# Gate logits of a routed expert layer from one pass over weights of 16 columns, six matrix products for a block in place of nine

## The chip, the cores and the metric

The kernel runs on one core of one Trainium2 chip. The metric is the time on the device in microseconds (us); lower is better. Times are medians of several executions, and one further execution was taken with the hardware profiler.

## The reference

The program is three layers one behind the other. The attention runs over 32 (batch, head) pairs with 768 tokens each; then comes a layer of eight experts, whose routing weights are made from gate logits by an exponential and eight rounds of normalisation over rows and columns; then a gated layer of two products. Only the middle one touches the change:

```python
def _moe_ref(x, w_gate, w1, w2):          # x: 3072 x 384, w_gate: 384 x 8
    logits = x @ w_gate
    logits = logits - logits.max()
    P = np.exp(logits)
    for _ in range(8):
        P /= P.sum(1, keepdims=True) + 1e-09
        P /= P.sum(0, keepdims=True) + 1e-09
        P *= N / E
    out = np.zeros((N, D), dtype=np.float32)
    for e in range(E):
        h = np.maximum(x @ w1[e], 0.0)
        ye = h @ w2[e]
        out += P[:, e:e + 1] * ye
    return out.astype(np.float32)
```

## The kernel before

Big matrix products are made in the type float32r, which TensorE takes in one product, from operands that are split into a high half (the value rounded to that type) and a low half (what the rounding left). A full product is then three: high by high, high by low, low by high. `PARTS = ((0, 0), (0, 1), (1, 0))` names them as (half of the weights, half of x). With the depth of 384 in three pieces of 128 (`KC` = 3) that makes nine matrix products of 384 columns for each output tile of a block of `TB` = 384 tokens. The 3072 tokens are eight such blocks, 0 to 7.

The program has two parts. In the first (the attention) the loop `for p in BODIES` goes over 24 pairs of (batch half, chunk of 128 tokens), and each body writes out by hand the order in which TensorE works: level products (L418, L428, L432, in the wait chain called `level_y` and `level_x`), the chain of the recurrence (L444, L456, L465, L473, L483 to L491), and between them eight slots, filled by the table `slots(p)`. A slot holds a tile of the expert layer's first product (`early_products`, L200), a turn of a finished tile of x (L499), or, always in slot 6, the gate logits: at p = 4, 7, ..., 19 the products of block 0 to 5 (`logit_products`, L509), and in the body behind each (p = 5, 8, ..., 20) their turn (`logit_flip`, L518). The products leave the logits of a block as 8 rows by 384 tokens in a bank of the accumulator memory (tile `bank`); VectorE copies them to `logit_a` (L826); the turn makes three tiles of 128 tokens by 8 experts of them with TensorE's transpose; and ScalarE copies these to `logit` (L641). TensorE, and every other engine, does its instructions in program order and waits on counters (semaphores) of the others. Since the accumulator banks of the slots are shared, the first product of a slot waits for the copy of the slot before the last.

The second part begins at about 606 us with the last six tiles of x. There the gate logits of blocks 6 and 7 are made in the same way (`logits_t`, L1219; `logits`, L1228; VectorE's copy L1445, ScalarE's copy L1353). The tile `gated`, in whose first rows that copy lands, shares its memory with `h_raw` and is shown under that name. Then come the maximum (L1502, L1256, L1504, L1260, L1506), the exponential (L1373) and the eight rounds of normalisation (VectorE L1511 to L1529 with one TensorE product each, L1328). TensorE fills the time with more tiles of the first expert product (L200), whose weights GpSimd (POOL) splits in L254. From 665 us on TensorE does the expert products one behind the other (L1292, L1321).

The gate weights are split once, by VectorE in `gate_split`, ahead of body p = 3.

Of the kernel before, what the change touches and what calls it, by code (L numbers as in the profile page):

```python
# [23 lines left out]
F32 = mybir.dt.float32  # L24
F32R = mybir.dt.float32r
F16 = mybir.dt.float16
BF16 = mybir.dt.bfloat16
ALU = mybir.AluOpType
# [3 lines left out]
P = 128  # L32
# [4 lines left out]
TB = 384  # L37
SINKHORN = 8
IDENT, UPPER, FIRST_T, LEVEL = 0, 1, 2, 2
PARTS = ((0, 0), (0, 1), (1, 0))  # L40
# [14 lines left out]
def wait(eng, sem, value):  # L55

    if isinstance(value, int) and value <= 0:
        return
    eng.wait_ge(sem, value)
# [41 lines left out]

def build(nc, kq_rows, kv_cols, beta_cols, w_gate, w1, w2, w_in, w_out, masks, out):
    NG, NCH, _, _, GH, D = kv_cols.shape
    S = NCH * P
    HS = beta_cols.shape[2]
    DM = w_gate.shape[0]
    KC = DM // P
    E, F = w1.shape[0], w1.shape[2]
# [10 lines left out]
    PASSES = early_passes(E * NH)  # L119
    EARLY_OF = [(i, hn, b, f) for i, (hn, blocks) in enumerate(PASSES) for b in blocks for f in range(FC)]  # L120
    PASS_FIRST = [FC * sum(len(blocks) for _, blocks in PASSES[:i]) for i in range(len(PASSES) + 1)]
    EARLY = len(EARLY_OF)
    IN_ATTENTION = (PAIRS - EARLY_FROM) * UPS
# [6 lines left out]
    with ExitStack() as top:  # L130
        def sb(name, shape, dt=F32, ctx=top):
            return ctx.enter_context(nc.sbuf_tensor(name, shape, dt))
# [4 lines left out]
        bank = top.enter_context(nc.psum_tensor("bank", [P, 8, 512], F32))  # L137


        ident = sb("ident", [P, P])  # L140
# [3 lines left out]
        x_early = sb("x_early", [P, 2, KC, EARLY_TOK], F32R)  # L144
# [2 lines left out]
        route = sb("route", [P, NT, E])  # L147
        logit = sb("logit", [P, NT, E])
        gate_raw = sb("gate_raw", [P, KC, E])
        gate_hl = sb("gate_hl", [P, 2, KC, E], F32R)  # L150
        rowsum = sb("rowsum", [P, NT])
        colsum = sb("colsum", [P, E])
        top1 = sb("top1", [P, 4])
# [22 lines left out]
        pe_xx, act_hi, dve_lo, dve_gate = map(sem, ("pe_xx", "act_hi", "dve_lo", "dve_gate"))  # L176
        pe_lt, dve_lt, pe_logit, act_logit = map(sem, ("pe_lt", "dve_lt", "pe_logit", "act_logit"))
# [34 lines left out]
        def early_store(sp, n):  # L212
            _, hn, blk, f = EARLY_OF[n]
            sp.wait_ge(act_e, n + 1)
            sp.dma_start(h_early[hn, blk, f, :, :], h_out[:, n % RING, :]).then_inc(st_h[n % RING], 16)
# [42 lines left out]
        with ExitStack() as at:  # L258
# [29 lines left out]
            logit_a = sb("logit_a", [P, TB], ctx=at)  # L288
# [59 lines left out]
            with nc.Block() as block:  # L348
# [47 lines left out]
                def _(pe):  # L396
# [106 lines left out]
                    def logit_products(b, to):  # L503

                        pe.wait_ge(dve_t, TT * (b + 1))
                        pe.wait_ge(dve_gate, 2)
                        for n, (a, c) in enumerate(PARTS):
                            for kc in range(KC):
                                m = pe.matmul(bank[0:E, to, 0:TB], gate_hl[:, a, kc, :],  # L509
                                              x_early[:, c, kc, b * TB:(b + 1) * TB], start=n + kc == 0,  # L510
                                              stop=n == len(PARTS) - 1 and kc == KC - 1)
                        m.then_inc(pe_lt, 1)

                    def logit_flip(b, to):

                        pe.wait_ge(dve_lt, b + 1)
                        for t in range(TT):
                            m = pe.transpose(bank[:, to, t * E:(t + 1) * E], logit_a[0:E, t * P:(t + 1) * P],  # L518
                                             ident[0:E, 0:E])
                        m.then_inc(pe_logit, 1)  # L520

                    def body(p):
                        ser, dbl, pre = pair(p), pair(p + 1), pair(p + 2)

                        def early(at, parts=range(9)):

                            if (item := slots(p)[at]) is None:
                                if -1 <= p < EARLY_FROM and at < 4:
                                    for _ in range(BUSY):
                                        pe.matmul(bank[:, BE + 1, 3 * P:4 * P], ident16[:, :], ident16[:, :],  # L530
                                                  start=True, stop=True)
                                return
                            if 0 in parts and (last := slot_before(p, at)) is not None:
                                done = {"up": act_e, "turn": dve_t, "logit": dve_lt, "flip": act_logit}[last[0]]
                                pe.wait_ge(done, last[1] + 1)
                            if item[0] == "up":
                                early_products(pe, item[1], BE + at % 2, parts)
                            elif item[0] == "turn":
                                turn_early(item[1], BE + at % 2)
                            elif item[0] == "logit":  # L540
                                logit_products(item[1], BE + at % 2)
                            else:
                                logit_flip(item[1], BE + at % 2)
# [168 lines left out]
                def _(dve):  # L712
# [109 lines left out]
                    def logits_out(b, at):  # L822
                        dve.wait_ge(pe_lt, b + 1)

                        wait(dve, pe_logit, b)
                        dve.tensor_copy(logit_a[0:E, :], bank[0:E, at, 0:TB]).then_inc(dve_lt, 1)  # L826

                    def gate_split():
                        dve.wait_ge(ld_gate, 16)
                        dve.tensor_copy(gate_hl[:, 0, :, :], gate_raw[:, :, :]).then_inc(dve_gate, 1)  # L830
                        dve.wait_ge(dve_gate, 1)
                        dve.tensor_tensor(gate_hl[:, 1, :, :], gate_raw[:, :, :], gate_hl[:, 0, :, :].bitcast(F32),
                                          ALU.subtract).then_inc(dve_gate, 1)

                    def body(p):
                        late, ser, dbl, pre, nrm = pair(p - 1), pair(p), pair(p + 1), pair(p + 2), pair(p + 3)

                        def early(at):

                            item = slots(p)[at]  # L840
                            if item is not None and item[0] == "turn":
                                turned_low(item[1], BE + at % 2)
                            if item is not None and item[0] == "logit":
                                logits_out(item[1], BE + at % 2)
# [47 lines left out]
                    for p in BODIES:  # L892
                        if p == -1:
                            dve.wait_ge(act_id, 1)
                        if p == EARLY_FROM - 1:
                            gate_split()
                        body(p)
# [110 lines left out]
        sig, gated = h_raw[:, 0:2, :], h_raw[:, 2:4, :]  # L1008
        w1_next = w1_raw[len(PASSES) % 2]
        w2_next = w_raw[:, 1 - len(PASSES) % 2, :].rearrange("p (k n) -> p k n", k=FC)  # L1010
        BL, BM, BL_T = 4, 5, 6
        logit_t = gated[0:E, :, :]
        out_t = out.rearrange("(t p) n -> p t n", p=P)
        EARLY_UNITS = {(hn, b) for hn, blocks in PASSES for b in blocks}
        HALVES = E * NH + NQ
# [3 lines left out]
        def x_at(c, kc, first, n):  # L1019

            if first < EARLY_TOK:
                return x_early[:, c, kc, first:first + n]
            return x_late[:, c, kc, first - EARLY_TOK:first - EARLY_TOK + n]
# [48 lines left out]
        with nc.Block() as block:  # L1072
# [132 lines left out]
            def _(pe):  # L1205
# [8 lines left out]

                def logits_t(b):
                    pe.wait_ge(dve_lo, TT * (b + 1) - ET)
                    for n, (a, c) in enumerate(PARTS):
                        for kc in range(KC):
                            m = pe.matmul(bank[0:E, BL_T + b % 2, 0:TB], gate_hl[:, a, kc, :],  # L1219
                                          x_at(c, kc, b * TB, TB), start=n + kc == 0,  # L1220
                                          stop=n == len(PARTS) - 1 and kc == KC - 1)
                    m.then_inc(pe_lt, 1)

                def logits(b):
                    pe.wait_ge(dve_lt, b + 1)
                    wait(pe, act_logit, b)
                    for t in range(TT):
                        m = pe.transpose(bank[:, BL, t * E:(t + 1) * E],  # L1228
                                         logit_t[:, b % 2, t * P:(t + 1) * P], ident[0:E, 0:E])
                    m.then_inc(pe_logit, 1)  # L1230

                def early(n):
# [9 lines left out]
                turn(21)  # L1242
                early(BEFORE_MAX[1])
                logits_t(6)
                turn(22)
                turn(23)
                early(BEFORE_MAX[2])
                logits(6)
                early(BEFORE_MAX[3])
                logits_t(7)  # L1250
                early(BEFORE_MAX[4])
                logits(7)
# [73 lines left out]
                for n in range(SINKHORN):  # L1326
                    pe.wait_ge(dve_sink, 3 + 8 * n + 4)
                    pe.matmul(bank[:, BM, 0:NT * E], ones[:, :], route.rearrange("p t e -> p (t e)"),  # L1328
                              start=True, stop=True).then_inc(pe_sink, 1)
# [105 lines left out]
            def _(dve):  # L1435
# [6 lines left out]

                def logits_out(b):
                    dve.wait_ge(pe_lt, b + 1)
                    dve.tensor_copy(logit_t[:, b % 2, :], bank[0:E, BL_T + b % 2, 0:TB]).then_inc(dve_lt, 1)  # L1445

                for t in range(18, 22):
                    turned_low(t)
# [59 lines left out]
                for n in range(SINKHORN):  # L1508
                    at = 3 + 8 * n
# [62 lines left out]
```

## Time and profile before

| | us |
|---|---|
| median of 3 runs (lowest, highest) | 2451.62 (2451.11, 2452.88) |
| the profiled execution, its own time | 2452.09 |
| its span in the profile | 2450.3 |
| TensorE busy with products | 2401.2 (98%) |
| VectorE, ScalarE, GpSimd busy | 1005.2, 659.3, 823.8 |

The span is the time from the first to the last instruction that the profile shows. The records of products overlap: each is shown from its start to its modelled end, so the cost of a product in a row of them is the distance from one start to the next, not the duration of a record. In the timeline a row merges like instructions: start, length from the first start to the last end, engine, line, operation, operands, count, and in brackets the idle time before it.

### The profile page before, as it was taken

The page shows a single profiled execution, that of the slowest core. Times are in us where ns is not written, and L with a number is a line of the kernel's source. Part 1 is how long each engine was busy: PE and PEld are TensorE (multiplying, and loading weights), DVE is VectorE, ACT ScalarE, POOL GpSimd, SP SyncE. Part 2 cuts the span into 40 slices and gives each one's busy share as a digit, 9 for nine tenths or more (in the row PEclk, how much of TensorE's full clock was granted, in tenths as well). Part 3 has the DMA queues.
Part 4 walks back from the last instruction along what each step waited for, and adds up shares of the span by engine and source line. Part 5 has one row for each costly group of instructions (what it writes and reads, how often), then busy time and mean ns, then how long its engine had stood idle before and what let it go on. Part 6 is the DMA issues. An engine that isn't in the chain of part 4 may idle for free.

```text
span 2450.3 us, 41885 instructions
## 1 busy us (share of the span) xinstructions
PE 2401.2 (98%) x17603; PEld 2329.4 (95%) x17603; DVE 1005.2 (41%) x2165; ACT 659.3 (27%) x1445; POOL 823.8 (34%) x831
## 2 busy tenths in 40 slices
PE   5999999999899999999999999999999999999999
PEld 4888888888899999999999999999999999999999
DVE  4866666664533333333333333333333343333332
ACT  3444444444321112111111111111111123222222
POOL 4655454542331333312302311321230413453432
PEclk9999999999999999999999999999999999999999
DMA  2233333322311111101110110110111100000001
GB/s 98 73 119 111 112 110 116 108 90 95 116 65 46 33 52 65 52 2 51 52 39 14 52 39 14 52 52 3 50 52 39 52 27 14 14 27 1 1 20 59
DMA packets 83963, 134.01 MB, mean 55 GB/s; under 512 B 5568, under 2 KB 62144, under 8 KB 83776
## 3 DMA queue, kind: packets, MB, share of 16 engines
q1 hardware_dynamic: 83776, 131.33, 16.2%
q8 instruction: 140, 2.29, 0.4%
q14 instruction: 47, 0.39, 0.0%
HBM read 98.28 MB, written 33.03 MB: 54 GB/s over the span
## 4 chain that ended last, share of the span: by engine, by line
PE 74%; DVE 1%; issue 0%; ACT 0%
PE bank L1321 41%; PE bank L1292 32%; PE bank L200 1%; PE bank L1268 0%; DVE rowsum L1513 0%; PE bank L1328 0%; PE bank L1219 0%; DVE route L1529 0%; PE bank L1211 0%; DVE route L1517 0%; DVE rowsum L1511 0%; ACT h_out L210 0%; DVE rowsum L1515 0%; DVE colsum L1521 0%; PE bank L1228 0%
## 5 line engine op out<-in xcount | busy, mean ns | idle before, releaser
L1321 PE MATMUL bank<-w_hl,h_hl 128*128 128x384 f32 x5760 | 1018.2, 334 | 0.0
L1321 PEld LDWEIGHTS bank<-w_hl,h_hl 128*128 128x128 f32 x5760 | 1000.2, 188 | 0.0
L1292 PE MATMUL bank<-x_early,w_hl 128*128 128x384 f32 x3024 | 539.1, 334 | 0.7 <-ACT h_out L210 0.7
L1292 PEld LDWEIGHTS bank<-x_early,w_hl 128*128 128x128 f32 x3024 | 525.1, 188 | 1.0 <-issue 1.0
L1173 POOL TENSOR_TENSOR h_hl<-h_raw,h_hl 128x384 fp32r<-128x384 f32 x144 | 141.8, 1015 | 951.7 <-ACT h_hl L1391 951.7
L1399 ACT ACTIVATE h_hl<-bank 128x384 fp32r<-128x384 f32 x368 | 181.1, 492 | 907.4 <-PE bank L1292 907.4
L1464 DVE SCALAR_TENSOR_TENSOR h_hl<-bank,h_hl 128x384 fp32r<-128x384 f32 x368 | 205.0, 557 | 412.2 <-ACT h_hl L1399 412.2
L1486 DVE SCALAR_TENSOR_TENSOR x_sum<-bank,route,x_sum 128x384 f32<-128x384 f32 x288 | 177.9, 618 | 391.0 <-PE bank L1321 391.0
L200 PE MATMUL bank<-x_early,w_hl 128*128 128x384 f32 x1296 | 287.2, 354 | 0.4 <-ACT h_out L210 0.4
L1292 PE MATMUL bank<-x_late,w_hl 128*128 128x384 f32 x1440 | 256.6, 334 | 0.0
L1292 PEld LDWEIGHTS bank<-x_late,w_hl 128*128 128x128 f32 x1440 | 250.1, 188 | 0.0
L1197 POOL TENSOR_TENSOR h_hl<-h_raw,h_hl 128x384 fp32r<-128x384 f32 x128 | 129.2, 1013 | 299.6 <-ACT h_hl L1409 299.6
L200 PEld LDWEIGHTS bank<-x_early,w_hl 128*128 128x128 f32 x1296 | 217.6, 190 | 6.7 <-issue 6.0
L618 ACT CAST xx<-bank 128x512 f16<-128x512 f32 x240 | 131.5, 592 | 121.9 <-PE bank L432 120.6
L754 DVE TENSOR_TENSOR yp<-bank,mask 128x256 f16<-128x256 f32 x288 | 112.3, 417 | 107.3 <-PE bank L418 105.2
L1476 DVE TENSOR_TENSOR h_raw<-bank,h_raw 128x384 f32<-128x384 f32 x128 | 71.3, 557 | 168.1 <-ACT h_raw L1418 121.5
L1143 POOL TENSOR_TENSOR w_hl<-w_raw,w_hl 128x1536 fp32r<-128x1536 f32 x39 | 136.6, 3503 | 2.6
L1418 ACT ACTIVATE h_raw<-bank 128x384 f32<-128x384 f32 x128 | 63.0, 492 | 265.4 <-PE bank L1292 265.4
L958 POOL TENSOR_TENSOR a_r<-lp,mask 128x256 f16<-128x256 f32 x96 | 70.0, 729 | 166.6 <-DVE lp L738 166.1
L1391 ACT CAST h_hl<-h_raw 128x384 fp32r<-128x384 f32 x144 | 63.3, 510 | 208.6 <-PE bank L1321 201.2
L254 POOL TENSOR_TENSOR w_hl<-w_raw,w_hl 128x512 fp32r<-128x512 f32 x63 | 79.9, 1279 | 98.9 <-ACT w_hl L249 98.1
L210 ACT ACTIVATE h_out<-bank 128x384 f32<-128x384 f32 x144 | 70.7, 491 | 157.6 <-PE bank L200 157.6
(125 smaller groups left out, 1914.3 us busy)
## 6 DMA issues: line engine op xcount, KB each, us to landing
w_raw<-in_moe_w SPq DMA_DIRECT2D x52, 768.0 KB, 6.3
h_early<-h_out SPq DMA_DIRECT2D x144, 192.0 KB, 1.9
h_raw<-h_early SPq DMA_DIRECT2D x36, 768.0 KB, 4.5
kq_t<-in_kq_rows SPq DMA_DIRECT2D x48, 256.0 KB, 2.7
kv<-in_kv_cols SPq DMA_DIRECT2D x24, 384.0 KB, 3.5
out<-x_sum SPq DMA_DIRECT2D x6, 576.0 KB, 3.0
w_raw<-in_moe_w_in SPq DMA_DIRECT2D x4, 768.0 KB, 4.3
w_raw<-in_moe_w_out SPq DMA_DIRECT2D x4, 768.0 KB, 4.4
```

Source lines behind the costliest of these rows:

```text
L200: last = pe.matmul(bank[:, b, 0:TB], w1_hl[i % 2][:, a, kc, f * P:(f + 1) * P], x_early[:, c, kc, blk * TB:(blk + 1) * TB], start=m == 0, ...
L254: pool.tensor_tensor(w1_hl[i % 2][:, 1, kc, :], w1_raw[i % 2][:, kc, :], w1_hl[i % 2][:, 0, kc, :].bitcast(F32), ALU.subtract).then_inc(po ...
L618: act.copy(grown(c, lev), b_grown(a, lev)).then_inc(act_xx_lev[a], 1)
L754: dve.tensor_tensor(blocks(yp[:, a, lev - 1, :, :], lev, 0), b_lev(a, 0, lev), keep.to_broadcast([P, GH, P >> (lev + 1), 1 << lev]), ALU.m ...
L1143: pool.tensor_tensor(dst[:, 1, :, :], raw[:, :, :], dst[:, 0, :, :].bitcast(F32), ALU.subtract).then_inc(pool_w, 1)
L1173: pool.tensor_tensor(h_hl[:, s % 2, 1, f, :], h_raw[:, f, :], h_hl[:, s % 2, 0, f, :].bitcast(F32), ALU.subtract).then_inc(pool_hlo, 1)
L1197: pool.tensor_tensor(h_hl[:, s % 2, 1, f, :], gated[:, n % 2, :], h_hl[:, s % 2, 0, f, :].bitcast(F32), ALU.subtract).then_inc(pool_lo, 1)
L1292: m = pe.matmul(bank[:, f, 0:TB], w1_hl[hn % 2][:, a, kc, f * P:(f + 1) * P], x_at(c, kc, b * TB, TB), start=n + kc == 0, stop=n == len(PA ...
L1321: m = pe.matmul(bank[:, 4 + t, 0:DM], h_hl[:, s % 2, a, f, t * P:(t + 1) * P], w2_hl[hn % 2][:, c, f, :], start=n + f == 0, stop=n == len( ...
L1399: act.activation(h_hl[:, s % 2, 0, f, :], bank[:, f, 0:TB], ACT.Relu).then_inc(act_h, 1)
L1464: dve.scalar_tensor_tensor(out=h_hl[:, s % 2, 1, f, :], in0=bank[:, f, 0:TB], scalar=0.0, in1=h_hl[:, s % 2, 0, f, :].bitcast(F32), op0=AL ...
L1486: dve.scalar_tensor_tensor(out=dst, in0=bank[:, 4 + t, 0:DM], scalar=route[:, b * TT + t, hn // NH:hn // NH + 1], in1=dst, op0=ALU.mult, o ...
```

## The change

The gate's high and low halves now stand side by side as 16 weight columns, so one product with a piece of x gives both halves' logits as 16 rows. A block takes six products (high and low half of x, three pieces each) where it took nine. Rows 0 to 7 are x times the gate's high half, rows 8 to 15 x times its low half. The product of both low halves, which was left out, is now part of it. VectorE copies 16 rows in place of 8. The turn is no longer TensorE's transpose: it is an ordinary float32 product of the 16 rows with the new tile `fold` (16 by 8, two identities one over the other), which turns and adds the two halves in one. VectorE makes `fold` with one more instruction in `gate_split`, and the counter `dve_gate` that the products wait for is asked for 3 in place of 2.

```diff
-        gate_hl = sb("gate_hl", [P, 2, KC, E], F32R)
+        gate_hl = sb("gate_hl", [P, KC, 2 * E], F32R)
+        fold = sb("fold", [2 * E, E])
...
                     def logit_products(b, to):
                         pe.wait_ge(dve_t, TT * (b + 1))
-                        pe.wait_ge(dve_gate, 2)
-                        for n, (a, c) in enumerate(PARTS):
+                        pe.wait_ge(dve_gate, 3)
+                        for c in range(2):
                             for kc in range(KC):
-                                m = pe.matmul(bank[0:E, to, 0:TB], gate_hl[:, a, kc, :],
-                                              x_early[:, c, kc, b * TB:(b + 1) * TB], start=n + kc == 0,
-                                              stop=n == len(PARTS) - 1 and kc == KC - 1)
+                                m = pe.matmul(bank[0:2 * E, to, 0:TB], gate_hl[:, kc, :],
+                                              x_early[:, c, kc, b * TB:(b + 1) * TB], start=c + kc == 0,
+                                              stop=c == 1 and kc == KC - 1)
                         m.then_inc(pe_lt, 1)
...
                     def logit_flip(b, to):
                         pe.wait_ge(dve_lt, b + 1)
                         for t in range(TT):
-                            m = pe.transpose(bank[:, to, t * E:(t + 1) * E], logit_a[0:E, t * P:(t + 1) * P],
-                                             ident[0:E, 0:E])
+                            m = pe.matmul(bank[:, to, t * E:(t + 1) * E], logit_a[0:2 * E, t * P:(t + 1) * P],
+                                          fold[:, :], start=True, stop=True)
                         m.then_inc(pe_logit, 1)
...
-                        dve.tensor_copy(logit_a[0:E, :], bank[0:E, at, 0:TB]).then_inc(dve_lt, 1)
+                        dve.tensor_copy(logit_a[0:2 * E, :], bank[0:2 * E, at, 0:TB]).then_inc(dve_lt, 1)
...
+                        dve.tensor_tensor(fold[:, :], ident[0:2 * E, 0:E], ident[0:2 * E, E:2 * E], ALU.add
+                                          ).then_inc(dve_gate, 1)
```

The second part has the same two edits in `logits_t` and `logits`, and in VectorE's copy `logits_out`.

Nothing changes its place. On TensorE, in slot 6 of body p = 4 (block 0), the rows before are:

```order
317 L200 MATMUL bank<-x_early,w_hl 128x384 x3
318 L509 MATMUL bank<-x_early,gate_hl 8x384 x9
319 L432 MATMUL bank<-xx,yp 128x64 x8
320 L483 MATMUL bank<-z,kb 128x96 x2
321 L488 MATMUL bank<-state,kq_t 128x96
```

and in the changed kernel, whose line numbers are one higher here:

```order
317 L201 MATMUL bank<-x_early,w_hl 128x384 x3
318 L510 MATMUL bank<-x_early,gate_hl 16x384 x6
319 L433 MATMUL bank<-xx,yp 128x64 x8
320 L484 MATMUL bank<-z,kb 128x96 x2
321 L489 MATMUL bank<-state,kq_t 128x96
```

Nine products with 8 output rows have become six with 16, between the same neighbours. In slot 6 of body p = 5 (the turn of block 0) TensorE has before:

```order
377 L418 MATMUL bank<-xx,a_r 128x64 x8
378 L200 MATMUL bank<-x_early,w_hl 128x384 x3
379 L518 MATMUL bank<-ident,logit_a 128x8 x3
380 L432 MATMUL bank<-xx,yp 128x64 x8
381 L488 MATMUL bank<-state,kq_t 128x96
```

and in the changed kernel:

```order
377 L419 MATMUL bank<-xx,a_r 128x64 x8
378 L201 MATMUL bank<-x_early,w_hl 128x384 x3
379 L519 MATMUL bank<-fold,logit_a 128x8 x3
380 L433 MATMUL bank<-xx,yp 128x64 x8
381 L489 MATMUL bank<-state,kq_t 128x96
```

The program still has three instructions there, which read `fold` in place of `ident` and are products, no transposes.

## Rows read from the trace of the kernel before

**Rows 1.** The page, part 1: busy time, share of the span, instructions

```profile
PE 2401.2 (98%) x17603; PEld 2329.4 (95%) x17603; DVE 1005.2 (41%) x2165; ACT 659.3 (27%) x1445; POOL 823.8 (34%) x831
```

**Rows 2.** Waits of PE in the whole span: us in total, times, longest

```profile
PE bank L405 <- DMA kq_t<-in_kq_rows: 13.8, 1, 13.8
...
PE bank L1328 <- DVE route L1517: 6.8, 3, 3.6
PE bank L418 <- ACT xx L618: 6.8, 27, 0.7
```

**Rows 3.** Busy time of PE, PEld, DVE, ACT, POOL, PE's clock, by stretch

```profile
98.00:605.00 507.00, 499.21 (x6010) 443.61 (x6009) 335.35 (x915) 231.79 (x537) 241.58 (x370) 1.00 0.33 107
605.00:628.00 23.00, 21.68 (x136) 18.81 (x135) 4.95 (x11) 9.41 (x21) 9.66 (x4) 1.00 0.30 104
628.00:663.00 35.00, 28.18 (x152) 27.23 (x151) 24.16 (x64) 10.91 (x23) 9.64 (x7) 0.95 0.38 128
663.00:2450.00 1787.00, 1782.63 (x10309) 1781.76 (x10308) 577.45 (x1001) 371.42 (x795) 512.41 (x350) 1.00 0.11 36
```

**Rows 4.** Instructions on tile gate_hl: ns min/median/max, first and last start

```profile
L509 PEld LDWEIGHTS bank<-x_early,gate_hl x54: 87/88/88, 139.3 to 514.9; 128*8 128x8 f32 x54
L509 PE MATMUL bank<-x_early,gate_hl x54: 331/334/340, 139.5 to 515.1; 128*8 128x384 f32 x54
...
L1219 PE MATMUL bank<-x_late,gate_hl x18: 332/338/340, 613.4 to 620.7; 128*8 128x384 f32 x18
```

**Rows 5.** Timeline of PE around the products of block 0

```profile
138.90 0.77 PE L200 MATMUL bank<-x_early,w_hl 128*128 128x384 f32 x3
139.51 1.72 PE L509 MATMUL bank<-x_early,gate_hl 128*8 128x384 f32 x9
141.07 0.41 PE L432 MATMUL bank<-xx,yp 128*128 128x64 f16 x8
```

**Rows 6.** The chain that ended last, one tile of L1292 with 128-column weights

```profile
741.02 6.24 PE bank L1292 x36
```

**Rows 7.** Timeline of PE around the turn of block 0

```profile
164.63 0.77 PE L200 MATMUL bank<-x_early,w_hl 128*128 128x384 f32 x3
165.33 0.35 PE L518 MATMUL bank<-ident,logit_a 8*128 8x8 f32 x3
165.61 0.41 PE L432 MATMUL bank<-xx,yp 128*128 128x64 f16 x8
```

**Rows 8.** Timeline of PE: ordinary float32 products (L465: four; L1260: one)

```profile
153.06 1.07 PE L465 MATMUL bank<-z,lp 128*128 128x48 f32 x8
153.97 0.28 PE L418 MATMUL bank<-xx,a_r 128*128 128x64 f16 x4
...
626.26 0.38 PE L1260 MATMUL bank<-top,ones 1*128 1x1 f32 x2
626.57 1.86 PE L200 MATMUL bank<-x_early,w_hl 128*128 128x384 f32 x9
```

**Rows 9.** Line L1260, its weight loads: ns min/median/max

```profile
L1260 PEld LDWEIGHTS bank<-top,ones x2: 181/182/184, 626.3 to 626.4; 1*128 1x128 f32 x2
```

**Rows 10.** Timeline of DVE and PE behind the products of block 0

```profile
141.27 0.55 DVE L826 COPY logit_a<-bank 8x384 f32<-8x384 f32 x1 [0.66 <-PE bank L509]
141.85 0.71 DVE L747 STREAM_TRANSPOSE xx<-xx 128x512 f16<-128x512 f16 x1
...
144.25 0.41 PE L418 MATMUL bank<-xx,a_r 128*128 128x64 f16 x8
```

**Rows 11.** Groups by line: a DVE copy of the same width on 128 rows

```profile
L1496 DVE COPY x_sum<-bank 128x384 f32<-128x384 f32 x18 | 10.0, 555 | 17.5 <-PE bank L1321 17.5
```

**Rows 12.** Timeline of DVE where the gate is split

```profile
98.12 0.18 DVE L832 TENSOR_TENSOR gate_hl<-gate_raw,gate_hl 128x24 fp32r<-128x24 f32 x1
...
98.50 0.76 DVE L754 TENSOR_TENSOR yp<-bank,mask 128x256 f16<-128x256 f32 x2 [0.20 <-PE bank L418]
```

**Rows 13.** Timeline of DVE and PE at the maximum over all logits

```profile
623.22 0.35 DVE L1502 TENSOR_REDUCE top<-logit 128x1 f32<-128x192 f32 x1 [1.61 <-ACT logit L1353]
...
624.47 0.27 PE L1256 MATMUL bank<-ident,top 128*1 128x128 f32 x1
```

**Rows 14.** Timeline of DVE, POOL and PE in the sixth round of normalisation

```profile
652.47 3.23 DVE L1513 TENSOR_SCALAR rowsum<-rowsum 128x24 f32<-128x24 f32 x1
...
653.65 2.02 POOL L1182 MEMSET x_last<- 128x2304 f32 x1
...
656.48 0.59 PE L1328 MATMUL bank<-route,ones 128*128 128x192 f32 x2 [3.60 <-DVE route L1517]
656.78 5.00 PE L200 MATMUL bank<-x_early,w_hl 128*128 128x384 f32 x18
```

More of the change, by code:

```diff
@@ L825, in logits_out @@
                         wait(dve, pe_logit, b)
-                        dve.tensor_copy(logit_a[0:E, :], bank[0:E, at, 0:TB]).then_inc(dve_lt, 1)
+                        dve.tensor_copy(logit_a[0:2 * E, :], bank[0:2 * E, at, 0:TB]).then_inc(dve_lt, 1)
                     def gate_split():
                         dve.wait_ge(ld_gate, 16)
-                        dve.tensor_copy(gate_hl[:, 0, :, :], gate_raw[:, :, :]).then_inc(dve_gate, 1)
+                        dve.tensor_copy(gate_hl[:, :, 0:E], gate_raw[:, :, :]).then_inc(dve_gate, 1)
                         dve.wait_ge(dve_gate, 1)
-                        dve.tensor_tensor(gate_hl[:, 1, :, :], gate_raw[:, :, :], gate_hl[:, 0, :, :].bitcast(F32),
+                        dve.tensor_tensor(gate_hl[:, :, E:2 * E], gate_raw[:, :, :], gate_hl[:, :, 0:E].bitcast(F32),
                                           ALU.subtract).then_inc(dve_gate, 1)
+                        dve.tensor_tensor(fold[:, :], ident[0:2 * E, 0:E], ident[0:2 * E, E:2 * E], ALU.add
+                                          ).then_inc(dve_gate, 1)
                     def body(p):
@@ L1011, in build @@
         BL, BM, BL_T = 4, 5, 6
-        logit_t = gated[0:E, :, :]
+        logit_t = gated[0:2 * E, :, :]
         out_t = out.rearrange("(t p) n -> p t n", p=P)
@@ L1216, in logits_t @@
                     pe.wait_ge(dve_lo, TT * (b + 1) - ET)
-                    for n, (a, c) in enumerate(PARTS):
+                    for c in range(2):
                         for kc in range(KC):
-                            m = pe.matmul(bank[0:E, BL_T + b % 2, 0:TB], gate_hl[:, a, kc, :],
-                                          x_at(c, kc, b * TB, TB), start=n + kc == 0,
-                                          stop=n == len(PARTS) - 1 and kc == KC - 1)
+                            m = pe.matmul(bank[0:2 * E, BL_T + b % 2, 0:TB], gate_hl[:, kc, :],
+                                          x_at(c, kc, b * TB, TB), start=c + kc == 0,
+                                          stop=c == 1 and kc == KC - 1)
                     m.then_inc(pe_lt, 1)
@@ L1227, in logits @@
                     for t in range(TT):
-                        m = pe.transpose(bank[:, BL, t * E:(t + 1) * E],
-                                         logit_t[:, b % 2, t * P:(t + 1) * P], ident[0:E, 0:E])
+                        m = pe.matmul(bank[:, BL, t * E:(t + 1) * E], logit_t[:, b % 2, t * P:(t + 1) * P],
+                                      fold[:, :], start=True, stop=True)
                     m.then_inc(pe_logit, 1)
@@ L1444, in logits_out @@
                     dve.wait_ge(pe_lt, b + 1)
-                    dve.tensor_copy(logit_t[:, b % 2, :], bank[0:E, BL_T + b % 2, 0:TB]).then_inc(dve_lt, 1)
+                    dve.tensor_copy(logit_t[:, b % 2, :], bank[0:2 * E, BL_T + b % 2, 0:TB]).then_inc(dve_lt, 1)
                 for t in range(18, 22):
```

## The prediction

> **What bounds the kernel now.** I read the page's busy times first, to see which engine is full: TensorE (PE), at 98% of the span, with the next engine at 41% [rows 1]. Then the waits of PE, to see whether the rest of the span is spent waiting where the change stands. It is not: the longest is one wait of 13.8 us for the first load, before the attention has begun; 6.8 us lie in the rounds of normalisation, and 6.8 us are spread over 27 short waits of L418 for ScalarE [rows 2]. Then busy times by stretch, to see whether PE is the bound in each of them: 499.21 of 507 us in the attention's full stretch, 21.68 of 23 where the last logits are made, 28.18 of 35 in the rounds of normalisation, 1782.63 of 1787 in the expert products [rows 3]. So PE in program order is the path almost everywhere, and what a block's products and turn cost on PE, from their first start to the start of the next group, goes into the end nearly one for one. Last I read the timeline of PE at a block's products and at its turn, for those distances.
>
> **The products: three fewer for each block.** There are 54 in the attention and 18 behind it, so 72 for eight blocks [rows 4]; 48 stay. The record of one is 334 ns long, but records overlap, so I take distances: nine start at 139.51 and the next group at 141.07, which is 1.56 us or 0.173 us for each [rows 5]. This is also the pace of the expert products, 36 in 6.24 us, whose weights have 128 columns [rows 6]. From this follows the answer on the wider weights: with 8 columns a weight load takes 88 ns [rows 4], and even 128 columns don't change the pace, so 16 can't. The pace comes from the 384 columns that stream through, and these stay. Three products fewer are 3 x 0.173 = 0.52 us less for each block.
>
> **The turn: three transposes become three float32 products.** Today's turn takes from 165.33 to 165.61, 0.28 us [rows 7]. The three products by `fold` have no row of their own. The nearest rows are ordinary float32 products that are also narrow: `product` (L465) issues four and shows eight records, L1260 issues one and shows two [rows 8]. So an ordinary float32 product runs as two pairs of weight load and product, and the turn becomes six pairs where it has three. Prices: L465's eight take from 153.06 to 153.97, 0.114 us a pair, with 48 columns; L1260's two take 0.31 us, 0.155 us a pair, with one column and the same PE state around it (float32r products before and behind) [rows 8]. From below I bound a pair with what a transpose pair takes today, 0.28/3 = 0.093 us. Six pairs are then 0.68 us, with bounds 0.56 and 0.93. I take 0.68: in L465 as in the new turn several stand in a row, so that all loads but the first can hide, while a lone product pays its entry on two pairs only. The turn gets dearer by 0.68 - 0.28 = 0.40 us (0.28 to 0.65).
>
> The Trainium skill says otherwise. "TensorE: Matmul & The Clock Gate", Terms, calls the transpose mode four times faster for FP32, and "FP8 and Floating Point Precision", TensorE Precision Notes, gives true FP32 four passes. The trace has two records for such a product, which doesn't say what goes on within one. Leaving the transpose mode would by that rule turn 0.28 us into 1.12 us as an estimate, and each block would lose 0.32 us in all, 2.6 us over the program.
>
> **What else is touched.** VectorE's copy has 16 rows in place of 8. It takes 0.55 us with 8 [rows 10], and the same width with 128 rows takes 555 ns [rows 11], so nothing changes. Behind it on VectorE the transpose L747 waits for the products today; with them 0.52 us shorter, copy and transpose end 0.52 us earlier, and PE, which needs that transpose at L418, comes 0.52 us earlier too. It had ended at 142.56 for a start at 144.25 [rows 10], so 1.7 us of cover stays. The new VectorE instruction is shorter than the 0.18 us of L832, and VectorE then idles 0.20 us for PE's L418 [rows 12]; it lies in that gap. If it didn't, it would cost 0.2 us once. The products wait for a third count that stands 41 us before they start (98.5 against 139.51), so that wait is free. At block 7 the turn's extra 0.40 us moves ScalarE's copy and the maximum L1502, and PE's next steps with them: L1502 ends at 623.57 and PE asks for it at 624.47 [rows 13], so its cover of 0.9 us stays as it is. Everything behind is started from PE, so the DVE and GpSimd instructions of the rounds keep their offsets.
>
> **The sum.** A block: -0.52 + 0.40 = -0.12 us. Eight blocks: -1.0 us (bounds: 8 x (0.28 - 0.52) = -1.9 and 8 x (0.65 - 0.52) = +1.0). The profiled execution's own 2452.09 us becomes 2451.1. It lies 0.47 us above the median, so for the median it is 2451.62 - 1.0 = 2450.7 us, a ratio of 1.000. A change under 0.2% (4.9 us) can't be told from none here, and the three runs themselves spread over 1.8 us.
>
> **The rivals.**
> *The weight loads of the turn don't hide behind each other.* L1260's load takes 182 ns [rows 9]; if each of the six pairs pays it in full, the turn is 1.09 us, a block loses 0.81 - 0.52 = 0.29 us, and the kernel 2.3 us: 2453.9. The sign turns where a pair costs more than (0.52 + 0.28)/6 = 0.133 us, which lies between the two rows, 0.114 and 0.155. For it: L1260's pairs are beyond that point. Against: L465's loads have all 128 rows and columns, take as long, and still go at 0.114. Chance 0.15. The skill's rule of four would land beside it, at 2454.2.
> *The turn costs what it costs today*, because products of 8 columns vanish behind the wait at its front (PE should have started the turn 0.18 us earlier by its own pace, 164.63 + 3 x 0.173 = 165.15 against 165.33 [rows 7]). Then all of 8 x 0.52 = 4.2 us stays: 2447.4. Against it are the doubled records. Chance 0.07.
> *A collision in the rounds of normalisation goes another way.* VectorE's L1513 took 3.23 us in the sixth round, until GpSimd's memset had ended; PE waited 3.60 us, and its next 18 products took 5.00 us [rows 14] where 17 distances of 0.173 and one record of 0.33 make 3.3 (the granted clock of that stretch is 0.95 [rows 3]). One more of those costs 3.6 + 1.7 = 5.3 us: 2456.9, slower by 0.22%. It needs the offset between the VectorE chain and GpSimd's splits to move by some tenths of a us, while both hang on the same PE order behind block 7's turn. The same mechanism can also take such a wait away (2446.3). Chance 0.03 each.
>
> **How the numbers follow.** The forecast, the sum within its own bounds (2449.2 to 2453.0 with the runs' spread), has 0.72; the rivals 0.15, 0.07, 0.03 and 0.03. The range goes from 2448.4 to 2454.0: it takes in the first rival and part of the second. Faster by over 0.2% is only the collision that goes away (0.03), slower by over 0.2% only the added one (0.03); all else is within 0.2%, 0.94.
>
> **What would show it.** In the profile of the changed kernel: six products of `gate_hl` from start to next group in 1.04 us; the turn with six records, 0.6 to 0.9 us to the next group; as many PE records as before in all (24 products fewer, 24 pairs more); PE's waits and the three long VectorE instructions of the rounds at the same rounds; a start of the expert products about 1 us earlier, with all behind it unchanged. It would be wrong if the turn had three records, if a pair cost above 0.133 us, or if the waits of L1328 summed to other than 6.8 us.

## The result

The changed kernel takes 2460.01 us (median of 7 runs, 2459.62 to 2463.19) against 2451.89 us for the kernel before (7 runs, 2451.11 to 2452.88): a ratio of 1.0035, interval [1.0024, 1.0047]. It is slower by 8.1 us. The prediction was 2450.7 us within 2448.4 to 2454.0, with 0.94 on no change that can be told.

The products of block 0 in the profile of the changed kernel, in PE's timeline:

```profile
138.41 0.77 PE L201 MATMUL bank<-x_early,w_hl 128*128 128x384 f32 x3
139.01 1.20 PE L510 MATMUL bank<-x_early,gate_hl 128*16 128x384 f32 x6
140.05 0.41 PE L433 MATMUL bank<-xx,yp 128*128 128x64 f16 x8
```

From 139.01 to 140.05 are 1.04 us, as forecast, for 1.56 before [rows 5]. The turn of block 0, in the same view:

```profile
163.61 0.77 PE L201 MATMUL bank<-x_early,w_hl 128*128 128x384 f32 x3
164.31 0.83 PE L519 MATMUL bank<-fold,logit_a 16*128 16x8 f32 x6
165.07 0.41 PE L433 MATMUL bank<-xx,yp 128*128 128x64 f16 x8
```

It has six records and takes 0.76 us to the next group (0.28 before [rows 7]; the forecast was 0.68 within 0.56 to 0.93). A block gains 0.52 - 0.48 = 0.04 us, so all eight gain 0.3 us. The attention and the rounds of normalisation lost nothing. PE's waits are those of before [rows 2]:

```profile
PE bank L406 <- DMA kq_t<-in_kq_rows: 14.0, 1, 14.0
PE bank L419 <- DVE xx L748: 7.8, 5, 3.9
PE bank L1331 <- DVE route L1520: 6.8, 3, 3.6
PE bank L419 <- ACT xx L619: 6.5, 27, 0.7
```

The expert products even start 1.02 us earlier, at 664.88 for 665.90. That is no gain of the change: 0.49 us of it is there before the first gate product (L201 ahead of it starts at 138.41 for 138.90), and in the runs below the instructions of the kernel before reach this point anywhere between 664.8 and 665.9 us. The loss lies behind that point, where the diff edits nothing. Here is the chain that ended last, first of the changed kernel and then of the kernel before, in the same stretch; a row is start, length, what:

```profile
664.88 12.72 PE bank L1295 x72
677.60 12.51 PE bank L1324 x72
690.11 6.27 PE bank L1295 x36
696.38 12.51 PE bank L1324 x72
708.88 6.36 PE bank L1295 x36
```

```profile
665.90 12.72 PE bank L1292 x72
678.62 12.48 PE bank L1321 x72
691.10 6.24 PE bank L1292 x36
697.34 12.48 PE bank L1321 x72
709.82 6.24 PE bank L1292 x36
```

Each group got longer by a hair: 12.51 for 12.48, 6.27 for 6.24, and 6.36 for 6.24 in the group that starts at 708.88. From the start of this stretch to the end of the span it is 2458.2 - 664.88 = 1793.3 us for 2450.3 - 665.90 = 1784.4: 8.9 us lost. The page's groups say where, out<-in, count | busy us, mean ns (after, then before):

```profile
L1324 PE MATMUL bank<-w_hl,h_hl 128*128 128x384 f32 x5760 | 1020.7, 335 | 0.0
L1295 PE MATMUL bank<-x_early,w_hl 128*128 128x384 f32 x3024 | 541.3, 335 | 0.7 <-ACT h_out L211 0.7
L1295 PE MATMUL bank<-x_late,w_hl 128*128 128x384 f32 x1440 | 261.1, 339 | 0.0
```

```profile
L1321 PE MATMUL bank<-w_hl,h_hl 128*128 128x384 f32 x5760 | 1018.2, 334 | 0.0
L1292 PE MATMUL bank<-x_early,w_hl 128*128 128x384 f32 x3024 | 539.1, 334 | 0.7 <-ACT h_out L210 0.7
L1292 PE MATMUL bank<-x_late,w_hl 128*128 128x384 f32 x1440 | 256.6, 334 | 0.0
```

Half of it, 4.5 us, falls on the 1440 products that stream `x_late` past the weights `w1_hl`. The clock isn't the cause. The stretch is granted the full 2.4 GHz (1.00, the last number but two), and PE is busy all of it:

```profile
663.00:2450.00 1787.00, 1786.33 (x10280) 1785.76 (x10280) 575.95 (x997) 371.19 (x795) 512.51 (x350) 1.00 0.11 36
```

Read product by product, the starts in the trace show two patterns. In a group on `x_late` every product is slow; the distances repeat 177.5, 175.0, 180.0, 174.2 ns (mean 176.7) where all products before take 173.3. In the other groups only the first few are slow, behind a border, which is a place where the stage goes over from one pair of tiles (weights and moving tile) to the other. The mean distance from each start to the next, over the 55 borders from `x_early` (L1292, now L1295) to the products of `h_hl` (L1321, now L1324) between 667 and 1925 us, for the first eight products:

```
before  173.6 173.3 173.3 173.2 173.5 173.3 173.4 173.2
after   172.5 175.0 177.5 185.0 175.8 181.7 173.3 173.3
```

What moved is the place of the tiles. "Nothing changes its place" holds for the instructions, not for the memory. `fold` is 32 bytes in every partition, and it is allocated ahead of `pad` and of all tiles of the expert stage. `w1_hl` and `x_early` stand ahead of it. So the distance from them to `x_late`, `h_hl` and `w2_hl` grew by 32 bytes. In the kernel before, all five begin at 128 over a multiple of 256 bytes (`w1_hl` at 12416 and 24704, `x_early` at 36992, `x_late` at 111232, `h_hl` at 129664, `w2_hl` at 154240 and 166528). Every slice of them that a product reads begins a multiple of 256 bytes behind the start of its tile, so the places of the tiles are also those of the operands.

### The profile page after: what moved, and what is told of

The parts are those of the page before. It is cut to its first block, busy times and chain, and to the rows that moved or that the text cites. A ratio compares the mean times of both kernels' runs of the same rounds, so it can differ in the third digit from the quotient of the medians.

```text
span 2458.2 us, 41886 instructions
## 1 busy us (share of the span) xinstructions
PE 2409.1 (98%) x17603; PEld 2339.2 (95%) x17603; DVE 1006.2 (41%) x2166; ACT 659.4 (27%) x1445; POOL 823.8 (34%) x831
## 4 chain that ended last, share of the span: by engine, by line
PE 74%; DVE 1%; ACT 0%; issue 0%; ACTq 0%
PE bank L1324 41%; PE bank L1295 32%; PE bank L201 1%; PE bank L1271 0%; DVE rowsum L1516 0%; PE bank L1331 0%; DVE route L1532 0%; PE bank L1214 0%; PE bank L1222 0%; PE bank L1231 0%; ACT L1376 0%; DVE route L1520 0%; DVE rowsum L1514 0%; ACT h_out L211 0%; DVE rowsum L1518 0%
## 5 line engine op out<-in xcount | busy, mean ns | idle before, releaser
L1324 PE MATMUL bank<-w_hl,h_hl 128*128 128x384 f32 x5760 | 1020.7, 335 | 0.0
L1324 PEld LDWEIGHTS bank<-w_hl,h_hl 128*128 128x128 f32 x5760 | 1002.5, 188 | 0.0
L1295 PE MATMUL bank<-x_early,w_hl 128*128 128x384 f32 x3024 | 541.3, 335 | 0.7 <-ACT h_out L211 0.7
L1295 PEld LDWEIGHTS bank<-x_early,w_hl 128*128 128x128 f32 x3024 | 527.2, 188 | 1.0 <-issue 1.0
L201 PE MATMUL bank<-x_early,w_hl 128*128 128x384 f32 x1296 | 286.6, 354 | 0.4 <-ACT h_out L211 0.4
L1295 PE MATMUL bank<-x_late,w_hl 128*128 128x384 f32 x1440 | 261.1, 339 | 0.0
L1295 PEld LDWEIGHTS bank<-x_late,w_hl 128*128 128x128 f32 x1440 | 254.5, 188 | 0.0
L201 PEld LDWEIGHTS bank<-x_early,w_hl 128*128 128x128 f32 x1296 | 216.9, 190 | 6.7 <-issue 6.0
```

Of the source, the lines that this page charges most:

```text
L201: last = pe.matmul(bank[:, b, 0:TB], w1_hl[i % 2][:, a, kc, f * P:(f + 1) * P], x_early[:, c, kc, blk * TB:(blk + 1) * TB], start=m == 0, ...
L1295: m = pe.matmul(bank[:, f, 0:TB], w1_hl[hn % 2][:, a, kc, f * P:(f + 1) * P], x_at(c, kc, b * TB, TB), start=n + kc == 0, stop=n == len(PA ...
L1324: m = pe.matmul(bank[:, 4 + t, 0:DM], h_hl[:, s % 2, a, f, t * P:(t + 1) * P], w2_hl[hn % 2][:, c, f, :], start=n + f == 0, stop=n == len( ...
```

## The experiments

They were measured in three sets, each with the kernel before beside it, which had medians of 2451.89, 2451.66 and 2451.51 us. Theory A is that the place of the tiles costs the 8 us; theory B that the change's own products, or an offset they cause, cost it.

**Changed kernel, tiles on a multiple of 64 again.**

```diff
-        pad = sb("pad", [P, 16])
+        pad = sb("pad", [P, 24])
```

> The changed kernel with the unused tile pad 32 bytes longer, so that every tile allocated behind it (x_late, h_hl, w2_hl, x_sum) begins at a multiple of 64 bytes again, as in the kernel before. Theory A (the place of the tiles costs the 8 us: fold took 32 bytes per partition and moved them to 32 over a multiple of 64): groups of 36 products on x_late are back at 6.24 us, the expert stage is as before, and the time is that of before plus 8 x (0.76 - 0.28 - 0.52) = -0.3 us: about 2451.5. Theory B (the new products, the float32 turn or an offset in the rounds of normalisation cost it, by whatever way): stays at 2460, x_late groups at 6.36.

2457.23 us, before 2451.89: 1.0025 [1.0016, 1.0034]. Neither theory as written. The groups on `x_late` are back, the borders are not:

```profile
677.50 12.51 PE bank L1324 x72
690.01 6.27 PE bank L1295 x36
696.28 12.51 PE bank L1324 x72
708.78 6.24 PE bank L1295 x36
```

So a multiple of 64 is not enough, or the change itself slows the borders. The next run and those with `pad` changed by other amounts decide.

**Kernel before, moved as the change moves it** (the same edit in the kernel before, not one instruction changed).

> The kernel before with pad 32 bytes longer and nothing else: the later tiles lie where the change puts them. Theory A: slower by what the expert stage lost, 4.8 us on x_late (40 groups of 36, 6.36 for 6.24 us) and about 4 us at the borders between the two kinds of product: about 2460.7. Theory B: 2451.9, no change.

2460.38 us, before 2451.89: 1.0034 [1.0022, 1.0047]. It has the whole loss (+8.5 us) and the changed kernel's lengths in the chain to 0.01 us:

```profile
677.96 12.51 PE bank L1321 x72
690.47 6.27 PE bank L1292 x36
696.73 12.51 PE bank L1321 x72
709.24 6.36 PE bank L1292 x36
```

From the first product of the expert stage to the end of the span both kernels take 1793.3 us, where the kernel before takes 1784.4. Theory B falls for the loss in the changed kernel.

**Kernel before, `h_hl` alone moved.**

```diff
+        shift_a = sb("shift_a", [P, 8])
         h_hl = sb("h_hl", [P, 2, 2, FC, TB], F32R)
+        shift_b = sb("shift_b", [P, 8])
```

> The kernel before with 32 bytes put ahead of h_hl and 32 behind it, so that of the operands of the expert stage h_hl alone (weights of L1321) lies at 32 over a multiple of 64, and w2_hl, x_late, w1_hl, x_early at a multiple. Theory A1 (a product is slow when its weights and its moving operand lie differently, one at 0 and one at 32 over a multiple of 64, as w1_hl and x_late do after the change): all 5760 products of L1321 take 176.7 ns for 173.5: +18 us, about 2470. Theory A2 (the moving operand's place alone counts): all moving operands are at a multiple, so 2451.9.

2472.80 us, before 2451.89: 1.0086 [1.0073, 1.01], +20.9 us. `w2_hl` is 64 bytes from its old place, `x_late` in it. Now it is the products of `h_hl` (line 1323 here) that are slow throughout:

```profile
677.79 12.71 PE bank L1323 x72
690.51 6.26 PE bank L1294 x36
```

72 take 12.71 for 12.48 us. It needs both tiles: in the run before this one `h_hl` lies in this same place (129696), and in the run with 64 bytes below `w2_hl` does (154304), and in neither are these products slow throughout. So neither the place of the weights nor that of the moving operand alone (A2) does it. The expectation had nothing for the borders, which came on top of its 18 us.

**Kernel before, all operands of the stage moved by the same 32 bytes.**

```diff
+        shift = sb("shift", [P, 8])
         w1_hl = [sb(f"w1_hl{n}", [P, 2, KC, FH], F32R) for n in range(2)]
```

> The kernel before with 32 bytes put ahead of w1_hl, so that w1_hl, x_early, x_late, h_hl and w2_hl all lie at 32 over a multiple of 64. Theory A1 (only a difference between weights and moving operand costs): all are alike again, 2452 within 1 us, all groups at 6.24. Theory A2 (a moving operand at 32 is slow where it comes with w1_hl): x_early pays too, 4464 products of L1292 by 3.2 ns: +14 us, about 2466.

2452.08 us, before 2451.89: 1.0 [0.9992, 1.0009]. Every group is at 12.48 and 6.24:

```profile
690.01 6.24 PE bank L1293 x36
696.25 12.48 PE bank L1322 x72
708.73 6.24 PE bank L1293 x36
```

Tiles that begin 32 bytes off cost nothing, as long as all do. What costs is that they differ from each other (A1).

**Changed kernel, every tile behind `pad` in its old place.**

```diff
-        pad = sb("pad", [P, 16])
+        pad = sb("pad", [P, 8])
```

> The changed kernel with pad 32 bytes shorter, so that fold takes its room and all tiles behind pad (those of the attention, x_late, h_hl, w2_hl) lie exactly where the kernel before has them. Theory A (the change's own instructions cost or save next to nothing, and all else is the place of the tiles): before plus 8 x (0.76 - 0.28 - 0.52) = -0.3 us, 2451.6, and no slow products at the borders of the expert stage. Theory B (the run with 32 bytes more kept 5.3 us, because the change itself costs something in the expert stage): about 2457.

2452.21 us, before 2451.66: 1.0005 [0.9996, 1.0013], no difference that can be told. The chain has the lengths of before:

```profile
678.41 12.48 PE bank L1324 x72
690.89 6.24 PE bank L1295 x36
697.13 12.48 PE bank L1324 x72
709.61 6.24 PE bank L1295 x36
```

This is the change that the prediction priced; its profiled span is 2450.1 us for 2450.3, and its expert stage takes 1784.4 us, as before. The gain of 0.3 us that the distances give is smaller than what this comparison can tell.

**Kernel before, moved by 64 and by 128 bytes** (`pad` of 32 and of 48 columns).

> The kernel before with pad 64 bytes longer and nothing else, which is the layout that the changed kernel had with 32 bytes more. Theory A3 (the borders between the two kinds of product cost where the tiles behind pad lie otherwise than w1_hl and x_early over a multiple of 128 bytes or more): 83 + 82 + 40 borders with 27 ns each are +5.5 us, about 2457.4, x_late groups at 6.24 us. Theory B (it needs the change's instructions): 2451.9.

> The kernel before with pad 128 bytes longer. Theory A3a (the place over a multiple of 128 bytes counts): as before, 2451.9, no slow product. Theory A3b (a longer period, 256 or 512 bytes; in the kernel before all operands of the stage lie at 128 over a multiple of 512): the borders cost again, about 2457.4.

64 bytes: 2456.97 us, before 2451.66, 1.0022 [1.0013, 1.0031]. So the borders' +5.3 us need no instruction of the change. 128 bytes: 2456.24 us, 1.0018 [1.001, 1.0027]. A3a falls. In this one the groups on `x_late` are slow again, which is most of its loss, while of the first products behind a border from `x_early` three are slow, and by little (174.2, 174.2 and 175.0 ns):

```profile
696.74 12.48 PE bank L1321 x72
709.22 6.34 PE bank L1292 x36
715.56 12.50 PE bank L1321 x72
```

**Kernel before, moved by 256 and by 512 bytes** (`pad` of 80 and of 144 columns).

> The kernel before with pad 256 bytes longer. If the places of the operands count over a multiple of 256 bytes: as before, 2451.9, all products at 173.3 ns. If the period is 512 bytes or there is none: slow products at the borders or on x_late again, some 4 to 5 us as with 64 and 128 bytes, about 2456.5.

> The kernel before with pad 512 bytes longer. If the places count over a multiple of 512 bytes or less: as before, 2451.9. If it is the distance itself that counts, and no multiple: slower again, about 2456.5.

2451.26 us and 2451.39 us, before 2451.51: 0.9999 [0.999, 1.0008] and 1.0 [0.9991, 1.0009]. Of the moves tried, 256 bytes is the smallest that costs nothing, and 512 costs nothing either. So it is the place over a multiple of 256 bytes that counts, as far as the distances tried (32, 64, 128, 256 and 512 bytes) show.

**Six products, and the transpose kept.** The three transposes take 16 rows, and VectorE adds the halves in place of ScalarE's copy.

```diff
-                            m = pe.matmul(bank[:, to, t * E:(t + 1) * E], logit_a[0:2 * E, t * P:(t + 1) * P],
-                                          fold[:, :], start=True, stop=True)
+                            m = pe.transpose(bank[:, to, t * 2 * E:(t + 1) * 2 * E],
+                                             logit_a[0:2 * E, t * P:(t + 1) * P], ident[0:2 * E, 0:2 * E])
...
+                        dve.tensor_reduce(logit[:, b * TT:(b + 1) * TT, :],
+                                          bank[:, at, 0:TT * 2 * E].rearrange("p (t c e) -> p t e c", c=2, e=E),
+                                          AX.X, ALU.add).then_inc(act_logit, 1)
```

> Six products as in the change, but without fold: the turn stays TensorE's transpose, of 16 rows, and VectorE adds the halves as it copies the logits out of the bank (one TENSOR_REDUCE of 48 elements in place of ScalarE's copy). All tiles stay where the kernel before has them. Theory A: products 1.04 us for 1.56, turn 0.28 to 0.30 us, so 8 x -0.50 = -4.0 us: 2447.9. Rival (the reduction or the wait on VectorE comes into PE's way, or the transposes of 16 columns cost more): 2451 or more.

2447.30 us (2446.47 to 2447.85), before 2451.66: 0.9981 [0.9973, 0.999]. It beats both kernels, by 4.4 us and by 12.7 us; products and turn account for 8 x 0.52 = 4.2 us. The turn, in PE's timeline, and the reduction, in VectorE's:

```profile
163.96 0.35 PE L518 MATMUL bank<-ident,logit_a 16*128 16x16 f32 x3
164.24 0.41 PE L432 MATMUL bank<-xx,yp 128*128 128x64 f16 x8
...
164.49 0.17 DVE L823 TENSOR_REDUCE logit<-bank 128x24 f32<-128x48 f32 x1
```

Three records and 0.28 us, as with 8 rows; the 0.17 us on VectorE lie beside PE's work.

**The float32 turn alone.** The kernel before with nine products, and its transposes made as ordinary products by the identity of 8 rows.

```diff
-                            m = pe.transpose(bank[:, to, t * E:(t + 1) * E], logit_a[0:E, t * P:(t + 1) * P],
-                                             ident[0:E, 0:E])
+                            m = pe.matmul(bank[:, to, t * E:(t + 1) * E], logit_a[0:E, t * P:(t + 1) * P],
+                                          ident[0:E, 0:E], start=True, stop=True)
```

> The kernel before, all tiles in their place and nine products, with the turn alone made as an ordinary float32 product by the identity of 8 rows in place of a transpose. If a turn costs 0.76 us for 0.28 on PE and nothing hides it: 8 x 0.48 = +3.8 us, 2455.6. If the medians with fold and with the transpose of 16 rows (2452.21 and 2447.30) tell its whole price: +4.9 us, 2456.7. If part of it is hidden: under 2455.

2457.96 us (2455.26 to 2458.67, 9 runs), before 2451.51: 1.0023 [1.0013, 1.0033]. That is +6.4 us, more than any of the three expectations. The runs fall in two heaps: four at 2455.26 to 2455.92 with a mean granted clock of 0.997 or 0.998, and five at 2457.96 to 2458.67 with 0.996. The first heap lies 3.8 to 4.4 us above the kernel before, about the +3.8 us that the distances give. The second has 2.7 us more, and its profile shows from where. The turn of block 4 in PE's timeline, and the clock by stretch (third column from the end):

```profile
465.68 0.29 PE L418 MATMUL bank<-xx,a_r 128*128 128x64 f16 x4 [0.31 <-ACT xx L618]
466.17 0.29 PE L418 MATMUL bank<-xx,a_r 128*128 128x64 f16 x4 [0.20 <-ACT xx L618]
466.29 0.77 PE L200 MATMUL bank<-x_early,w_hl 128*128 128x384 f32 x3
466.99 0.83 PE L518 MATMUL bank<-ident,logit_a 8*128 8x8 f32 x6
467.75 0.52 PE L432 MATMUL bank<-xx,yp 128*128 128x64 f16 x8
468.08 0.72 PE L488 MATMUL bank<-state,kq_t 128*128 128x96 f32 x2
```

```profile
466.00:468.00 2.00, 1.83 (x20) 1.57 (x21) 1.93 (x5) 0.26 (x2) 1.92 (x3) 0.98 0.51 137
468.00:474.00 6.00, 6.00 (x35) 5.67 (x31) 1.01 (x4) 1.60 (x6) 1.81 (x4) 0.50 0.17 46
474.00:476.00 2.00, 2.00 (x26) 1.42 (x24) 0.63 (x3) 1.06 (x2) 0.00 (x0) 0.82 0.70 185
```

PE stood still twice, then did the narrow turn of 0.76 us, and from about 468 us on it was granted 0.50, the lower of its two levels (1.2 GHz), for some 7 us. The kernel before has the same two waits of 0.31 and 0.20 us ahead of this turn, from 464.34 us on, and there the clock stays at 1.00. The same two heaps stand in the runs of the other kernels with a float32 turn: with the tiles in the old place seven of 11 at 2451.3 to 2452.7 and four at 2454.1 to 2455.2 (0.996), in the changed kernel with `pad` 32 bytes longer seven of 11 at 2456.4 to 2457.5 and four at 2459.6 to 2459.9, and in the changed kernel itself one of seven, at 2463.19. So 14 of 38 runs with a float32 turn lie 2.0 to 3.2 us above the middle of the others of their kernel. Without it one of 162 does (2453.95 us, with all operands moved by 32 bytes), and no run of the kernel before is more than 1.4 us above its median. That the float32 turn brings this dip on is seen in these counts and in one profile; by what condition was not tried.

## Why the prediction was wrong

- **What bounds the kernel** was right: PE in program order, and the losses and gains on PE went into the end.
- **The products** were right: 1.04 us for six, and a weight load of 16 columns (94 ns for 88) hidden.
- **The turn** was sized too low, by 0.08 us: six pairs, as argued, at 0.76/6 = 0.127 us and not 0.114. The sum of a block is -0.04 us, not -0.12, which is 0.6 us over the program and not what made the prediction fail. The rival with unhidden weight loads (1.09 us) did not come about, nor the one with a turn as cheap as today's. "TensorE: Matmul & The Clock Gate", Terms, in the Trainium skill, calls the transpose mode four times faster for FP32, which as an estimate makes the turn 1.12 us. The trace doesn't agree: it shows 0.76 us, a factor of 2.7.
- **What else is touched** is the step that failed, and with it the forecast of the last paragraph, "with all behind it unchanged": the expert stage was put at no change, and it took 1793.3 us for 1784.4. The step went through instructions and waits, and left out that a new tile of 32 bytes moves every tile allocated behind it. The nine runs that move tiles or hold them show that this alone is the loss: without any change of instructions the move costs 8.5 us, and the change without the move 0.55 us, within an interval that takes in zero. None of the three signs of being wrong that the prediction names came up (the turn has six records, a pair is below 0.133 us, the waits are 6.8 us), and none of them looked at the pace of the expert products. That these start 1 us earlier, as forecast, is luck: the sum, with the turn as measured, gives 0.3 us.
- **How a move costs** is shown in part. Products are slow throughout when their weights and their moving tile begin 32 bytes apart over a multiple of 256 (`w1_hl` and `x_late`; in the run with `h_hl` moved 32 bytes from `w1_hl` and 32 from `w2_hl`, the products of L1321), or 128 apart (6.34 us for 36). At 64 apart they are not, once going. In both cases with 32 bytes the moving tile lies 32 bytes higher than the weights; the other way round was not tried. Where the stage goes over to a pair of tiles at another place, some of the first products are often slow, but not at each border: in the changed kernel the products of `h_hl` behind a group on `x_late` keep 173.3 ns from the first, and with a move of 64 bytes those on `x_late` do. No rule that covers all borders was found. Since the pace depends on two tiles at once, and the weights of the next product load while this one streams, a possible reason is that the two reads get in each other's way. A hint for it is in the gate's own products: their weight slices lie 32 or 96 bytes from `x_early` over a multiple of 256 in the changed kernel, but are 16 columns wide and not 128, and six took 1.04 us, 173 ns each. Still it is argued: no run took the overlap away. "TensorE: Matmul & The Clock Gate", Step-by-step, in the Trainium skill, says that loading the next weights takes nothing from the running product's reads, as TensorE has two read ports. Where the tiles lie alike the trace agrees: with weights of 128 columns, whose load takes 188 ns, a product takes 173 ns, as it does with weights of 8 columns. No run here bears it out for tiles that lie differently: 36 products took 6.36 us for 6.24 by place alone.
- **The collision rival** did not occur: the waits of L1331 are the same 6.8 us. Its prices were also added to the time before and not to the forecast; from 2450.7 us they would be 2456.0 and 2445.4, and the first of these is slower by 0.18%, not by over 0.2%. The upper end with the runs' spread, 2453.0 us, should be 2453.9 by the same reckoning as the lower one.
- **A cost nobody priced** is the clock: 14 of 38 executions with a float32 turn lose 2.0 to 3.2 us more. In the run with the turn alone these are five of nine, so they set its median, and most of the step from 3.8 to 6.4 us is theirs. In the other three kernels the median is that of an execution without it.

## What to carry to other kernels

A change that adds, drops or resizes a tile also moves the tiles allocated behind it, and in a stage where PE is full that may outweigh its instructions: here 32 bytes cost 8.5 us in some 10,000 products. Before comparing two versions, print the addresses of the stage's operands, keep those of weights and moving tiles alike over a multiple of 256 bytes, or give the new tile its room out of padding. And where a prediction says that a stage stays as it is, name a row of that stage whose change would contradict it. When narrow float32 data is only to be turned, stay with the transpose (three take 0.28 us, whether of 8 or 16 rows, and three float32 products 0.76) and let an engine with idle time do the sum.

## What the runs showed of the hardware

- The pace of float32r products of 128 by 128 by 384 depends on where their two operands lie to each other: 173.3 ns where both begin alike over a multiple of 256 bytes, and 176.7 ns at 32 bytes apart. Alike at 128 and alike at 160 over a multiple of 256 cost the same. Moving the later tiles by 256 or 512 bytes changes nothing, by 64 or 128 it costs 5.3 and 4.6 us.
- Behind a border between `x_early` and `h_hl` the slow products follow one fixed row, 175.0, 177.5, 185.0, 175.8, 181.7 ns, with moves of 32 and of 64 bytes, and then the pace is back at 173.3. The borders to and from `x_late` show, with these moves, only the last three of these or none, apart from the groups that are slow throughout.
- An ordinary float32 product is two pairs of weight load and product in the trace, 0.127 us a pair for weights of 16 rows by 128 columns and 8 columns moving. A transpose is one pair.
- Three narrow float32 products behind two short waits were followed by some 7 us at the lower clock, in an attention stretch that had kept the full one in the kernel before.
